# A mixture-of-experts stage on one core: where TensorE's step ends, and the order of work on the last tile

## The reference

```python
logits = np.einsum('bsd,de->bse', x, w_gate)
local_gate = 1.0 / (1.0 + np.exp(-np.einsum('bsd,de->bse', x, w_local).squeeze(-1)))
...
fresh_e = int(np.argmax(logits[b, s]))
if s == 0 or local_gate[b, s] < 0.5:
    e = fresh_e
else:
    e = prev_e if prev_e >= 0 else fresh_e
...
h = np.maximum(x[b, s] @ w1[e], 0.0)      # 512 -> 1024
out[b, s] = p[e] * (h @ w2[e])            # 1024 -> 512
```

## Time and profile before

| | us |
|---|---|
| median of 3 runs | 860.29 (860.20 to 860.36) |
| the profiled execution | 861.76 |
| its span, first to last instruction | 859.9 |
| PE busy in the span | 837.5 (97%) |
| DVE, ACT, POOL busy | 406.2, 339.0, 245.6 |
| mean granted TensorE clock | 0.994 of full |

### The profile page before, as it was taken

One profiled execution on the slowest core, in us unless ns is written; L12 is line 12 of the kernel. 1 busy time (PEld: TensorE's weight loads), 2 busy tenths in 40 slices (PEclk: granted clock), 3 DMA queues, 4 the chain that ended last, 5 costly groups with the idle time before them and its releaser, 6 DMA issues.

```text
span 859.9 us, 19730 instructions
## 1 busy us (share of the span) xinstructions
PE 837.5 (97%) x7380; PEld 724.1 (84%) x7381; DVE 406.2 (47%) x731; ACT 339.0 (39%) x752; POOL 245.6 (29%) x288
## 2 busy tenths in 40 slices
PE   7899999999999999999999999999999999999995
PEld 6899999799999998799989998888778888888884
DVE  5677777511255245335536744543873513422121
ACT  4677777411146135215513523531434423422120
POOL 5977878793000000000000000039252212221121
PEclk9999999999999999999999999999999999999997
DMA  6554443139332012002201202415341612211111
GB/s 170 133 140 117 114 118 99 53 122 26 1 97 63 13 53 67 29 5 82 62 1 62 62 25 94 152 36 193 124 142 59 226 37 85 105 39 34 43 51 32
DMA packets 36175, 68.04 MB, mean 79 GB/s; under 512 B 11352, under 2 KB 11480, under 8 KB 36120
## 3 DMA queue, kind: packets, MB, share of 16 engines
q1 hardware_dynamic: 26168, 44.90, 20.0%
q10 hardware_dynamic: 6512, 11.64, 4.5%
q0 software_dynamic: 3440, 10.75, 3.9%
HBM read 57.84 MB, written 9.98 MB: 79 GB/s over the span
## 4 chain that ended last, share of the span: by engine, by line
PE 90%; DVE 4%; ACT 2%; issue 2%; DMA 1%; POOL 1%; ACTq 0%; POOLq 0%; DVEq 0%
PE bank L1746 23%; PE bank L1748 22%; PE bank L1747 22%; PE bank L1686 4%; PE bank L1631 4%; PE bank L1656 4%; PE bank L1641 1%; PE bank L1955 1%; PE bank L1793 1%; DMA stage<-gate_rows 1%; PE bank L1619 1%; DVE stage L1209 1%; PE bank L1672 1%; PE bank L1822 1%; ACT stage L1014 1%
## 5 line engine op out<-in xcount | busy, mean ns | idle before, releaser
L1178 DVE SCALAR_TENSOR_TENSOR hid_lo<-bank,hid_hi 128x384 fp32r<-128x384 f32 x96 | 53.5, 557 | 210.0 <-ACT hid_hi L990 210.0
L1748 PE MATMUL bank<-uT_hi,W 128*128 128x384 f32 x384 | 129.6, 337 | 0.0
L1746 PE MATMUL bank<-uT_hi,W 128*128 128x384 f32 x384 | 129.4, 337 | 0.0
L1747 PE MATMUL bank<-uT_lo,W 128*128 128x384 f32 x384 | 128.9, 336 | 0.0
L990 ACT ACTIVATE hid_hi<-bank 128x384 fp32r<-128x384 f32 x96 | 46.9, 488 | 186.8 <-PE bank L1748 186.7
L1014 ACT ACTIVATE stage<-stage 128x512 f32<-128x512 f32 x135 | 84.6, 627 | 77.4 <-DVE stage L1209 70.9
L1746 PE MATMUL bank<-W,hid_hi 128*128 128x512 f32 x288 | 114.0, 396 | 0.2 <-DVE hid_lo L1178 0.2
L1748 PE MATMUL bank<-W,hid_lo 128*128 128x512 f32 x288 | 113.7, 395 | 0.0
L1747 PE MATMUL bank<-W,hid_hi 128*128 128x512 f32 x288 | 113.4, 394 | 0.0
L1209 DVE TENSOR_TENSOR stage<-rows,stage 128x512 f32<-128x512 f32 x135 | 89.0, 687 | 11.2 <-ACT stage L1014 8.5
L1746 PEld LDWEIGHTS bank<-uT_hi,W 128*128 128x128 f32 x384 | 72.2, 188 | 3.9
(11 more groups left out here) (305 smaller groups left out, 1544.4 us busy)
## 6 DMA issues: line engine op xcount, KB each, us to landing
rows<-in_moe_w SPq DMA_DIRECT2D x12, 1024.0 KB, 5.2
stage<-gate_rows ACTq DMA_DIRECT2D x38, 256.0 KB, 3.2
stage<-in_moe_w_ch SPq DMA_DIRECT2D x16, 512.0 KB, 4.6
qk_raw<-in_q SPq DMA_DIRECT2D x32, 144.0 KB, 3.6
vv<-in_v SPq DMA_DIRECT2D x32, 144.0 KB, 2.7
x_rows<-rows SPq DMA_DIRECT2D x6, 768.0 KB, 3.3
qk_raw<-in_k SPq DMA_DIRECT2D x30, 144.0 KB, 3.9
late_stage<-in_moe_w SPq DMA_DIRECT2D x4, 1024.0 KB, 6.6
```

Source lines behind the costliest of these rows:

```text
L1178: dve.scalar_tensor_tensor(out=hid_lo[:, n % 2], in0=bank[:, HB[n % 2], 0:TOK], scalar=0.0, in1=hid_hi[:, n % 2].bitcast(F32), op0=ALU.max ...
L1746: pe.matmul(dst, lhs_hi, rhs_hi, start=start, stop=False)
L1747: pe.matmul(dst, lhs_hi, rhs_lo, start=False, stop=False)
L1748: return pe.matmul(dst, lhs_lo, rhs_hi, start=False, stop=stop)
```

## The change

Four parts:

- On TensorE `step(i)` now ends behind the up products. It starts with the first four chunks (12 matmuls) of the down products of tile i-2, then come the table and the waits for `h_out`, for the rows of tile i+1 and for the weights, then the other four chunks, then the turns (`turns`) and the up products of tile i. The matmuls of all tiles but the last stand in the same order as before; what moves against them is the place of the waits, the table reads and the branches. The branches for tiles 18 to 25 are now a loop of two tiles a round, whose rounds are also gone through when `end` is already passed.
- For the last tile the order of matmuls is new: first half of the down products of tile `end`-1, the turns of `end`, second half of `end`-1, down products of `end`. These go to bank 0, so they don't wait for the `weigh` before. A new semaphore `b_half` tells ACT that the first half of `hT` may be overwritten.
- On DVE `h_lo_halves(i, 0)` comes before `weigh(i - 1)`.
- On POOL `gather(4)` comes behind the three `oh_p` instructions.

The three products no longer stand behind a gather. The diff, without the hunks that only create `b_half` and set `LAST_PRODUCTS = 0`:

```diff
@@ -439,15 +440,12 @@
-        def sure_steps(eng, step):
+        def expert_steps(eng, step):
+            end = load_last(eng)
             step(EARLY_T + 1, 1)
             with eng.Fori(EARLY_T // 2 + 1, FULL // 2) as n:
                 step(2 * n, 0)
                 step(2 * n + 1, 1)
-
-        def expert_steps(eng, step):
-            end = load_last(eng)
-            sure_steps(eng, step)
             with eng.Fori(FULL // 2, TILES // 2) as n:
                 for odd in range(2):
@@ -900,13 +899,13 @@
             pool.wait_ge(ids_ready, 1)
             scatter(0)
-            pool.wait_ge(xg_used, 3)
-            gather(4)
             pool.wait_ge(xT_out, 3)
             pool.wait_ge(oh_tile_ready, 1)
                 pool.tensor_tensor(oh_p[:, :, w, :], oh_tile[:, :, :], over_i(part[:, :]), ALU.mult)\
                     .then_inc(oh_p_ready, 1)
+            pool.wait_ge(xg_used, 3)
+            gather(4)
             scatter(1)
             pool.wait_ge(xg_used, 5)
@@ -1069,8 +1068,10 @@
             def hT_halves(i, g):
                 act.wait_ge(tr_done, 2 * i + g + 1)
-                act.wait_ge(b_done, i)
-                if g == 1:
+                if g == 0:
+                    act.wait_ge(b_half, i)
+                else:
+                    act.wait_ge(b_done, i)
                     act.wait_ge(xg_used, i + 3)
                 act.activation(by_half(hT_hi[:, 4 * g:4 * g + 4]), turned_half(g, H_COLS[g]), ACT.Copy)\
@@ -1452,11 +1453,11 @@
                                   hT_hi[:, 4 * g:4 * g + 4].bitcast(F32), ALU.subtract).then_inc(hT_out, 1)
-            def weigh(i):
+            def weigh(i, products=5):
                 dve.wait_ge(b_done, i + 1)
                 if not (isinstance(i, int) and i == 0):
                     dve.wait_ge(y_stored, 16 * i)
-                dve.tensor_tensor(y, bank[:, 5, 0:DM], slot_p[:, ds(i, 1)].to_broadcast([P, DM]), ALU.mult)\
+                dve.tensor_tensor(y, bank[:, products, 0:DM], slot_p[:, ds(i, 1)].to_broadcast([P, DM]), ALU.mult)\
                    .then_inc(y_out, 1)
@@ -1572,8 +1573,8 @@
                 with dve.If((todo & UP) != 0):
                     prepare(i, 0)
+                h_lo_halves(i, 0)
                 weigh(i - 1)
-                h_lo_halves(i, 0)
                 h_lo_halves(i, 1)
                 x_lo_halves(i + 2, par)
@@ -1588,7 +1589,7 @@
             piece_lo(1, 1, 2)
             piece_lo(1, 1, 3)
-            weigh(expert_steps(dve, step))
+            weigh(expert_steps(dve, step), LAST_PRODUCTS)
         @block.tensor
@@ -1917,13 +1918,15 @@
                 up_part(par, 1, range(1, KC))
-            def down_part(i, par, chunks):
+            def down_part(i, par, chunks, products=5, waits=True):
                 w_hi, w_lo = expert_part(par, 0), expert_part(par, 1)
                 for c in chunks:
-                    if c % 4 == 0:
+                    if waits and c % 4 == 0:
                         pe.wait_ge(hT_out, 2 * i + c // 4 + 1)
-                    mm = three(bank[:, 5, 0:DM], hT_hi[:, c], hT_lo[:, c], down_chunk(w_hi, c), down_chunk(w_lo, c),
-                               c == 0, c == NEC - 1)
+                    mm = three(bank[:, products, 0:DM], hT_hi[:, c], hT_lo[:, c], down_chunk(w_hi, c),
+                               down_chunk(w_lo, c), c == 0, c == NEC - 1)
+                    if c == NEC // 2 - 1:
+                        mm.then_inc(b_half, 1)
                 if c == NEC - 1:
                     mm.then_inc(b_done, 1)
@@ -1960,28 +1963,32 @@
                 pe.wait_ge(xT_out, i)
+            def x_ready(i):
+                pe.wait_ge(gathered, 16 * i)
+                pe.wait_ge(xT_out, i)
+
+            def turns(i):
+                turn_h_halves(i, 0)
+                turn_h_halves(i, 1)
+                turn_x_halves(i + 2)
+
             def step(i, x_par):
+                if isinstance(i, int) and i == EARLY_T + 2:
+                    down_part(i - 2, 0, range(6, NEC))
+                elif not (isinstance(i, int) and i == EARLY_T + 1):
+                    older = of_tile(i - 2)
+                    down_start(i - 2, *older, range(NEC // 2))
                 par, ord_ = of_tile(i)
                 pe.wait_ge(ew_lo, 2 * EP * ord_ + EP)
                     x_ready(i + 1)
                     settled(pe)
-                    turn_h_halves(i - 1, 0)
-                    turn_h_halves(i - 1, 1)
-                    turn_x_halves(i + 1)
+                    if not (isinstance(i, int) and i == EARLY_T + 2):
+                        down_part(i - 2, older[0], range(NEC // 2, NEC))
+                    turns(i - 1)
                 up_part(par, 0, range(KC), x_par)
                 up_part(par, 1, range(KC), x_par)
-                if isinstance(i, int) and i == EARLY_T + 1:
-                    down_part(i - 1, 0, range(6, NEC))
-                else:
-                    down_start(i - 1, *of_tile(i - 1), range(NEC))
-
-            def last_steps(i):
-                if i < TILES:
-                    with pe.If(end >= i):
-                        step(i, i % 2)
-                        last_steps(i + 1)
             turn_x(0)
@@ -2048,18 +2055,29 @@
             pe.wait_ge(tables_ready, 1)
             end = load_last(pe)
-            sure_steps(pe, step)
-            last_steps(FULL)
-            par, ord_ = of_tile(end)
-            pe.wait_ge(ew_lo, 2 * EP * ord_ + 2 * EP)
+            step(EARLY_T + 1, 1)
+            step(EARLY_T + 2, 0)
+            with pe.Fori(EARLY_T // 2, FULL // 2 - 2) as n:
+                step(2 * n + 3, 1)
+                step(2 * n + 4, 0)
+            step(FULL - 1, 1)
+            with pe.Fori(FULL // 2, TILES // 2) as n:
+                with pe.If(end >= 2 * n):
+                    step(2 * n, 0)
+                    with pe.If(end >= 2 * n + 1):
+                        step(2 * n + 1, 1)
+            older = of_tile(end - 1)
+            newest = of_tile(end)
+            pe.wait_ge(ew_lo, 2 * EP * older[1] + 2 * EP)
+            pe.wait_ge(hT_out, 2 * end)
+            down_part(end - 1, older[0], range(NEC // 2), waits=False)
+            pe.wait_ge(ew_lo, 2 * EP * newest[1] + 2 * EP)
             pe.wait_ge(h_out, 2 * end + 2)
             x_ready(end + 2)
             settled(pe)
-            turn_h_halves(end, 0)
-            turn_h_halves(end, 1)
-            turn_x_halves(end + 2)
-            pe.wait_ge(y_out, end)
-            down_part(end, par, range(NEC))
+            turns(end)
+            down_part(end - 1, older[0], range(NEC // 2, NEC), waits=False)
+            down_part(end, newest[0], range(NEC), LAST_PRODUCTS)
```

More of the change, by code:

```diff
@@ L410, in moe_kernel @@
         hT_out = sem("hT_out")
+        b_half = sem("b_half")
         b_done = sem("b_done")
@@ L488, in moe_kernel @@
         LAST_BANKS = (2, 3, 5)
+        LAST_PRODUCTS = 0
         EARLY = len(first_jobs)
```

## The result

| | median | runs | profiled execution | its span |
|---|---|---|---|---|
| before | 860.25 us | 859.75 to 860.36 | 861.76 us | 859.9 us |
| after | 866.28 us | 864.05 to 867.05 | 864.05 us | 862.2 us |

The ratio is 1.0067 (95% interval 1.0047 to 1.0087): 6 us slower. A second set of runs of the same changed kernel gave 1.0069 (1.0055 to 1.0082). The forecast was 3.2 us slower.

The account below looks back on a forecast made before the run. TensorE, 97% busy, was taken to bound the kernel through its waits and clock. Gains of 6.8 us against losses of 10.0 put the profiled 861.76 at 865.0, and 863.5 for the median; range 857.8 to 868.0.

Parts of the forecast that it names:

- Last tile, -6.2 predicted: At the last tile, the new order runs without gaps and at full clock, gaining 6.2 us (bounds 5.4 to 6.2).
- Before the loop, -0.6 predicted: Before the loop, `oh_p` starts earlier by 0 to 1.03 us and shortens TensorE's 1.25 us wait; gain 0.6 us.
- Ordinary steps, zero margin, nothing lost: At 12 of 16 row waits, margin 2.0 us less 1.5 and 0.45 leaves nothing, and nothing is lost.
- Three slower gathers, +1.5: The loop's first and last two gathers land in about 4.0 us, 0.5 us late each; loss 1.5 us together.
- Step 7, 3.9 and 0.7 for POOL's hold: Step 6's gather lands late beside two weight loads, 3.9 us; a DVE split holding POOL adds 0.7 us.
- The meeting stays: Weight loads move by the same 1.5 us as the gather of step 6, so the two still meet.
- The held gather of step 11, +1.7: At the next change of expert, a DVE split holds POOL's gather with no load; loss 1.7 us (bounds 0 and 2.0).
- That of step 5, 0: A split starts within 0.4 us of step 5's gather; loss taken as 0 (bounds 0 and 2.0).
- The clock, +2.2: Behind a stall over 4 us, TensorE's clock falls to 1.2 GHz; loss 2.2 us (bounds 0 and 3.4).
- The rival "only small waits are left": In the loop, gathered rows come in time and only small waits of 0.6 us remain; 854.1 us, chance 0.12.
- The rival of a negative margin in all steps: In 12 ordinary steps, landing to product takes 0.95 us, adding 0.5 us each, 6 us; 869.5 us, chance 0.12.
- The rival of the empty rounds: At the loop's end, three empty rounds fetch code, up to 6 x 3.35 us, net 16 to 18; 880 us, chance 0.04.

Follow-up runs that it names:

- e6: Changed kernel with weigh first in all tiles but the last, TensorE's row wait at the turns, and 12 more empty rounds; ratio to before 1.0063.
- e11: Changed kernel with POOL's gather ahead of its scatter, all waits at the turns, two table reads ahead of the loop; ratio to before 0.9930.
- e4: Kernel before with POOL's part alone, the gather of tile 4 behind the oh_p products; ratio to before 0.9967.
- e1: Changed kernel with weigh ahead of the first hT_lo split again in all tiles but the last; ratio to before 0.9958.
- e10: The changed kernel run again, unaltered; ratio to before 1.0069.
- e12: Changed kernel with each weight load in the loop moving only an eighth of its columns; ratio to before 1.0008.
- e2: Changed kernel with TensorE's wait for gathered rows alone moved back to the turns, weigh still late; ratio to before 0.9934.
- e8: Changed kernel with POOL alone reordered, gather ahead of scatter in each expert tile; ratio to before 0.9928.
- e9: Changed kernel with TensorE's waits for rows, hrow and weights all back at the turns, weigh still late; ratio to before 0.9927.
- e5: Kernel before with the late weigh alone, DVE running the first hT_lo split ahead of weigh; ratio to before 1.0018.
- e7: Changed kernel with weigh first in all tiles but the last and TensorE's row wait six products earlier; ratio to before 1.0008.

## Why the prediction was right, and where it was not

The forecast was 863.5 us, the result 866.28, within the range and on the side that was called likeliest. Point by point, in the profiled executions:

- **Last tile, -6.2 predicted.** From the first down product of tile 18 to the last product it is 843.27 to 855.16, 11.9 us, and was 18.0: -6.1. What I had put at nothing, the empty rounds and table reads, takes 0.34 us of idle time just ahead of it. As a whole it is -5.6 to -5.8. The step that failed in it is "I cost them at nothing": the lead of about 4 us was right, but three rounds (2.2 us) and two reads use all of it, as e6 and e11 show.
- **Before the loop, -0.6 predicted.** -1.5, by e4. The bound of 1.03 us was wrong, since it priced `oh_p`'s earlier start and not the DVE instruction that took 3.33 us beside it and takes 0.84 in the new order.
- **Ordinary steps, zero margin, nothing lost.** Right. `weigh` and the gather start 1.74 and 5.34 us behind the turns (712.77):

```profile
714.51 0.68 DVE L1460 TENSOR_TENSOR stage<-bank,slot_p 128x512 f32<-128x512 f32 x1
...
718.11 1.00 POOL L836 DMA_INDIRECT stage<-x_rows,gid_now  x1 [0.79 <-POOL gid_now L841]
```

  In e1 the gather starts 3.93 behind (658.40 to 662.33), so the delay is 1.4 us, 1.5 predicted. In most ordinary steps no wait is listed; a product of up to 0.49 instead of 0.39 us at the thirteenth place is all there is to see.
- **Three slower gathers, +1.5.** Nearly absent: steps 5 and 19 show 0.2 us of idle time each (0.21 and 0.41 in e10).
- **Step 7, 3.9 and 0.7 for POOL's hold.** 4.37 (4.05 in e10), so the sum was right. Its split was not: e12 gives 2.5 to the loads and 1.8 to the late weigh and the hold. "The meeting stays" came true, but not for the reason given: the held gather of step 5 moved the loads by 2 us more, and only the wait in step 6 brought the next gather back to them.
- **The held gather of step 11, +1.7.** 1.53 in step 12. Right. **That of step 5, 0.** Wrong: it was held for 3.02 us and cost 1.64 us in step 6. I had given it bounds of 0 and 2.0, and it took the upper part. This is the term that was most mis-sized.
- **The clock, +2.2.** 1.5. Right in kind.
- **The mechanism.** Right, with one part missing: the wait for `hrow` moved forward too. It costs nothing in the changed kernel, where the rows are later still, but 1.06 us show in e2.

From these the loop took 260.91 - 256.75 + 1.5 + 5.7 = 11.4 us more than before, 10.0 predicted. Idle time for rows is 7.5 of it and the clock 1.5. The rest, some 2.4 us, is weight loads that show behind each wait, two more waits of 0.2 us and up to 0.1 us in a step; I did not separate them. That gives +4.2 for the stretch, where +3.2 was forecast. The closeness of the sums is in part luck. Terms that were too high (the three slower gathers by 1.1, the clock by 0.7, steps 7 and 12 by 0.4) cancelled most of those that were too low (step 6 by 1.6, the small delays by 2.0). The timed runs say +6.0; both profiled executions of the changed kernel were the fastest of their sets, and their stretches agree, so the other 2 us lie in a part that the change does not touch or in executions that I have not seen. That is left open.

The chances as worked out in the prediction add up to 0.20, 0.24 and 0.56 for faster, same and slower; 0.19 and 0.57 are slips.

The rival "only small waits are left" (854.1) is near what e2, e8 and e9 (853.9 to 855.5 us) show once one of the two delays is taken back. The rival of a negative margin in all steps is not what happened: 11 of the 16 steps wait for nothing. The rival of the empty rounds was right in that they are not free, and wrong in its price, 0.73 us a round. The Trainium skill (Runtime: NRT & Kernel Launch, Instruction fetch mechanics) has a taken branch out of a window of two blocks of code wait for a fetch. The jumps of e6 over a pair of steps show no such wait. Whether their targets lay outside that window stands in no row, so this speaks against the rival, and not, as the prediction had it for the loop's branches, against the rule.

## What to carry to other kernels

Two edits that each take from the same slack must be priced together: 1.6 us and at most 1.2 us alone became 11 us in one kernel, because together they left nothing for gathers that a split holds and for the one transfer that lands late, and made a stall behind which the clock fell. A stall can also bring the next transfer back into the meeting that it had just escaped. When a wait is moved forward, write down every semaphore that moves with it, and look at what stands ahead of the awaited transfer in its issuing queue: here one moved line on POOL (gather before scatter) made both edits nearly free. A loop's empty rounds and a table read are free only where the sequencer has a lead, and each place has only one lead to spend.

## What the runs showed of the hardware

- A gather issued on POOL takes 1.00 us, and 2.8 to 3.1 us when a DVE split of 128x2048 (2.29 us, two inputs in SBUF) has started 0.1 to 0.35 us before it (the changed kernel, e2, e5, e9, e10 and e12). The one at the same place ahead of the loop was held in all 14 profiles (2.84 or 2.85 us). The Trainium skill (SBUF — State Buffer, SBUF: two separate sides) describes an exclusive lock for the length of an instruction between GpSimd, when it reads SBUF, and a DVE instruction with two inputs there. The trace agrees, with a hold that ends 0.9 us behind the split.
- The gather of step 6 lands 3.4 us after its start where that is 1.74 us ahead of two 1024 KB loads (e5), and 7.2 to 7.7 us after it where it is 0.4 us behind the first of them (before, e6, e7, e8).
- Granted clock: it stayed at 2.4 GHz behind waits of 1.3, 1.64 and 1.84 us, and was at 1.2 GHz for 3 to 4 us behind 3.43, 4.05 and 4.37 us. In the kernel before it fell behind 0.41 and 1.96 us with three turns between them. Behind 8.89 us it was at 1.2 GHz longer (0.76, 0.50 and 0.72 in 840 to 855 of e6).
- A branch of TensorE over the code of a pair of steps took 0.20 to 0.22 us, in 15 rounds in a row in e6. The one of 3.35 us in the earlier trace rows went over six written-out tiles and has no like in the changed kernel.
